# The second gate's products of a block in three bfloat16 parts instead of float32 (attention, a top-1 expert layer and a capacity expert layer on one core)

## What is computed

```python
attn = local_and_global_attention(q, k, v)            # 4 x 8 heads, 768 positions, 64 wide
x = attn rows                                          # 3072 tokens x 512
# first expert layer: one expert per token, only where x @ w_skip > 0
e = argmax(x @ moe_w_gate); g = softmax(x @ moe_w_gate)[e]
x[live] += g * (relu(x @ moe_w1[e]) @ moe_w2[e])       # 8 experts, 512 -> 1024 -> 512
# second expert layer: tokens are assigned by the sorted second gate's logits, at most 384 per expert
logits2 = x @ moe2_w_gate                              # 3072 x 8
assign greedily in falling order of logits2
out = relu(x @ moe2_w1[e]) @ moe2_w2[e]
```

## Time and profile before

| | |
|---|---|
| Time, median of 3 runs | 813.74 us (812.87 to 814.51) |
| Profiled execution's own time | 815.21 us |
| Its span in the trace | 813.5 us |
| TensorE matmul busy | 753.9 us, 93% of the span |
| VectorE busy | 537.1 us, 66% |
| ScalarE busy | 453.7 us, 56% |
| GpSimd (POOL) busy | 165.4 us, 20% |
| First experts in the trace | about 246 to 470 us |
| Mean granted clock of TensorE | 0.97 |

### The profile page before, as it was taken

The page is one execution under the profiler, slowest core; times in us unless marked ns, Lnnn a source line. Parts: engine busy times, 40 slices in busy tenths (PEclk is TensorE's granted clock), DMA queues, the critical chain, the costliest instruction groups (busy, mean ns, idle before and its releaser), DMA issues. The chain is left out here.

```text
span 813.5 us, 15742 instructions
## 1 busy us (share of the span) xinstructions
PE 753.9 (93%) x5590; PEld 675.1 (83%) x5590; DVE 537.1 (66%) x1463; ACT 453.7 (56%) x919; POOL 165.4 (20%) x184
## 2 busy tenths in 40 slices
PE   2899999999959999999999938999999999999997
PEld 2899999999928988899888825888888888888896
DVE  6877778777477778766666557766666767675420
ACT  3889888888525454554545303545554554536360
POOL 8100000000030222222221101141414141423321
PEclk9999999999959999999999957999999999999999
DMA  8998987986264666535763006768675777769861
GB/s 179 217 215 221 240 204 210 212 209 167 99 205 156 215 241 216 182 121 218 245 223 126 13 9 227 186 223 199 198 199 194 196 208 187 220 178 302 226 130 44
DMA packets 64106, 151.65 MB, mean 186 GB/s; under 512 B 12294, under 2 KB 15750, under 8 KB 64016
## 3 DMA queue, kind: packets, MB, share of 16 engines
q1 hardware_dynamic: 52512, 114.77, 48.3%
q0 software_dynamic: 11504, 35.72, 18.1%
HBM read 118.84 MB, written 16.67 MB: 167 GB/s over the span
## 5 line engine op out<-in xcount | busy, mean ns | idle before, releaser
L1817 PE MATMUL r_ph<-r_xh,r_w1h 128*128 128x384 f32 x256 | 90.6, 354 | 0.0
L1817 PE MATMUL r_ph<-r_xh,r_w1l 128*128 128x384 f32 x256 | 86.2, 337 | 0.0
L1817 PE MATMUL r_ph<-r_xl,r_w1h 128*128 128x384 f32 x256 | 85.8, 335 | 0.0
L592 ACT ACTIVATE pr<-pr,nmx 128x232 f32<-128x232 f32 (+1 forms) x192 | 79.9, 467 | 9.6 <-DVE nmx L685 9.6
L1098 PE MATMUL m_ph<-m_xh,m_w1h 128*128 128x224 f32 x288 | 80.9, 281 | 0.1
L1252 ACT ACTIVATE m_hh<-m_ph 128x224 fp32r<-128x224 f32 (+1 forms) x72 | 25.2, 350 | 97.9 <-PE m_ph L1098 93.9
L1098 PE MATMUL m_ph<-m_xh,m_w1l 128*128 128x224 f32 x288 | 79.1, 275 | 0.0
L1098 PE MATMUL m_ph<-m_xl,m_w1h 128*128 128x224 f32 x288 | 78.9, 274 | 0.0
L685 DVE CUSTOM_DVE_ANT_0 pr<-sc,bias 128x232 f32<-128x232 f32 (+1 forms) x192 | 65.0, 374 | 19.5 <-PE sc L466 17.5
L599 ACT ACTIVATE prt<-tp 128x384 f32<-128x384 f32 (+1 forms) x128 | 65.5, 537 | 22.0 <-PE tp L478 18.5
L1831 PE MATMUL r_py<-r_w2h,r_hh 128*128 128x512 f32 x192 | 76.1, 396 | 0.0
(11 more groups left out here) (298 smaller groups left out, 1960.5 us busy)
## 6 DMA issues: line engine op xcount, KB each, us to landing
r_w<-moe_w SPq DMA_DIRECT2D x64, 512.0 KB, 5.1
m_w<-moe_w SPq DMA_DIRECT2D x36, 512.0 KB, 5.9
row_buf<-moe_w SPq DMA_DIRECT2D x9, 2048.0 KB, 8.7
r_w2l<-r_w POOLq DMA_DIRECT2D x32, 512.0 KB, 4.9
k_raw<-kI SPq DMA_DIRECT2D x64, 208.0 KB, 7.2
q_raw<-qT SPq DMA_DIRECT2D x64, 192.0 KB, 7.6
vo<-vL SPq DMA_DIRECT2D x16, 384.0 KB
x_rows<-row_buf SPq DMA_DIRECT2D x4, 1536.0 KB, 6.6
```

Of the source, the lines that this page charges most:

```text
L592: nc.scalar.activation(pr[n % PRS][:, t, lo:CW], pr[n % PRS][:, t, lo:CW], ACT.Exp, bias=nmx[n % PRS][:, t:t + 1], scale=-1.0).then_inc(ex ...
L1817: last = nc.tensor.matmul(ph[m % 4][:, 0:CAP], w[:, c, m * P:(m + 1) * P], x[:, c, :], start=(c == 0 and a == 0), stop=(c == KC - 1 and a ...
```

## The change

The second gate's products of blocks 0 to 7 no longer read float32 rows and weights. The weights are split once into three bfloat16 parts (`split_gate2`, in VectorE's side work of block 0), which lie side by side as 24 columns. The turned rows of a block are split into three bfloat16 parts too: ScalarE writes the first (its copy now goes to `y_parts[0]`), VectorE subtracts it from the turned rows into `yt` (float32), ScalarE writes the second from `yt` for two chunks at once, and VectorE subtracts again into the third. All nine products are taken by 24 matmuls with 24 moving columns, accumulated over chunks and row parts, and VectorE sums the three groups of 8 columns. `Z_AT` becomes 2, 3, 4, 5: the wide copies and subtractions stand behind chunks 3 and 4, the products behind chunk 5 as before. TensorE's turns of chunk 2 and 3 now wait for VectorE's subtraction (`yt_low`) of chunk 0 and 1. The overflow block's own gate part stays float32.

```diff
+        wg2_parts, wg2_rest = sb("wg2_parts", [P, KC, 3, E], BF16), sb("wg2_rest", [P, KC, E])
+            y_parts = [tb(f"y_part{i}", [P, KC, WIDE1], BF16) for i in range(3)]
-            Z_AT, OVER_AT = (2, 3, 5), 3
+            Z_AT, OVER_AT = (2, 3, 4, 5), 3
+            def in_parts(k):
+                return isinstance(k, int) and k < E
+            def kept_before(k):
+                return 6 * k if isinstance(k, int) and k <= E else KC * k + (6 - KC) * E
 # TensorE, z_part
                             if c >= 2:
-                                pe.wait_ge(yt_kept, KC * k + c - 1)
+                                pe.wait_ge(yt_low if in_parts(k) else yt_kept, kept_before(k) + c - 1)
-                    else:
-                        pe.wait_ge(yt_kept, KC * k + KC)
+                    elif i == 3 and in_parts(k):
+                        pe.wait_ge(yt_kept, kept_before(k) + 6)
+                        pe.wait_ge(yt_low, kept_before(k) + 6)
                         for t in tiles(k):
                             r = rows_in(k, t)
                             for c in range(KC):
-                                last = nc.tensor.matmul(pt[0][0:r, BLK + t * E:BLK + (t + 1) * E], yt[:, c, t * P:t * P + r], wg2[:, c, :],
-                                                        start=(c == 0), stop=(c == KC - 1))
+                                for a in range(3):
+                                    last = nc.tensor.matmul(pt[0][0:r, BLK + t * 3 * E:BLK + (t + 1) * 3 * E], y_parts[a][:, c, t * P:t * P + r],
+                                                            wg2_parts[:, c].rearrange("p a e -> p (a e)"), start=(c == 0 and a == 0), stop=(c == KC - 1 and a == 2))
+                        last.then_inc(z_done, 1)
 # ScalarE, z_part
-                            nc.scalar.activation(yt[:, c, 0:W], pt[c % 2][:, BLK:BLK + W], ACT.Copy).then_inc(yt_kept, 1)
+                            dst = y_parts[0][:, c, 0:W] if in_parts(k) else yt[:, c, 0:W]
+                            nc.scalar.activation(dst, pt[c % 2][:, BLK:BLK + W], ACT.Copy).then_inc(yt_kept, 1)
+                    if i in (1, 2) and in_parts(k):
+                        two = slice(2 * i - 2, 2 * i)
+                        act.wait_ge(yt_low, kept_before(k) + 2 * i)
+                        nc.scalar.activation(y_parts[1][:, two, :], yt[:, two, 0:WIDE1], ACT.Copy).then_inc(yt_kept, 1)
 # VectorE, z_part
+                    if i < 2 and in_parts(k):
+                        for c in (2 * i, 2 * i + 1):
+                            dve.wait_ge(yt_kept, kept_before(k) + c + 1)
+                            v.tensor_tensor(yt[:, c, 0:WIDE1], pt[c % 2][:, BLK:BLK + WIDE1], y_parts[0][:, c, :], ALU.subtract).then_inc(yt_low, 1)
+                    if i in (1, 2) and in_parts(k):
+                        two = slice(2 * i - 2, 2 * i)
+                        dve.wait_ge(yt_kept, kept_before(k) + 4 + i)
+                        v.tensor_tensor(y_parts[2][:, two, :], yt[:, two, 0:WIDE1], y_parts[1][:, two, :], ALU.subtract).then_inc(yt_low, 1)
-                            last = v.tensor_copy(zo[s][0:r, t, :], pt[0][0:r, BLK + t * E:BLK + (t + 1) * E])
+                                parts = pt[0][0:r, BLK + t * 3 * E:BLK + (t + 1) * 3 * E].rearrange("p (a e) -> p e a", e=E)
+                                last = v.tensor_reduce(zo[s][0:r, t, :], parts, AX.X, ALU.add)
 # VectorE, ahead of the rest of count_extra
+                def split_gate2():
+                    link(v.tensor_copy(wg2_parts[:, :, 0, :], wg2[:]))
+                    link(v.tensor_tensor(wg2_rest[:], wg2[:], wg2_parts[:, :, 0, :], ALU.subtract))
+                    link(v.tensor_copy(wg2_parts[:, :, 1, :], wg2_rest[:]))
+                    link(v.tensor_tensor(wg2_parts[:, :, 2, :], wg2_rest[:], wg2_parts[:, :, 1, :], ALU.subtract))
```

More of the change, by code:

```diff
@@ L848, in build @@
             h_done, h_high, h_low, y_done, y_kept = (sem(x) for x in ("h_done", "h_high", "h_low", "y_done", "y_kept"))
-            yt_turned, yt_kept, z_done, z_kept = (sem(x) for x in ("yt_turned", "yt_kept", "z_done", "z_kept"))
+            yt_turned, yt_kept, yt_low, z_done, z_kept = (sem(x) for x in ("yt_turned", "yt_kept", "yt_low", "z_done", "z_kept"))
             gathered, scattered, z_scattered = ([sem(f"{x}{s}") for s in range(2)] for x in ("gathered", "scattered", "z_scattered"))
@@ L1081, in z_part @@
                             for c in range(KC):
-                                last = nc.tensor.matmul(pt[0][0:r, BLK + t * E:BLK + (t + 1) * E], yt[:, c, t * P:t * P + r], wg2[:, c, :],
-                                                        start=(c == 0), stop=(c == KC - 1))
+                                for a in range(3):
+                                    last = nc.tensor.matmul(pt[0][0:r, BLK + t * 3 * E:BLK + (t + 1) * 3 * E], y_parts[a][:, c, t * P:t * P + r],
+                                                            wg2_parts[:, c].rearrange("p a e -> p (a e)"), start=(c == 0 and a == 0), stop=(c == KC - 1 and a == 2))
+                        last.then_inc(z_done, 1)
+                    elif i == 3:
+                        pe.wait_ge(yt_kept, kept_before(k) + KC)
+                        for c in range(KC):
+                            last = nc.tensor.matmul(pt[0][:, BLK:BLK + E], yt[:, c, 0:P], wg2[:, c, :], start=(c == 0), stop=(c == KC - 1))
                         last.then_inc(z_done, 1)
@@ L1176, in _ @@
                 with pe.If(n < 1):
-                    for i in range(3):
+                    for i in range(4):
                         z_part(E - 1, 1, i)
@@ L1195, in _ @@
                         turn_limits()
-                    z_part(E, 0, 2)
+                    z_part(E, 0, 3)
                     with pe.If(n < 2):
@@ L1312, in z_part @@
                 def z_part(k, s, i):
-                    if i == 2:
+                    if i < 2 and in_parts(k):
[6 more added lines that the diff above has]
+                        v.tensor_tensor(y_parts[2][:, two, :], yt[:, two, 0:WIDE1], y_parts[1][:, two, :], ALU.subtract).then_inc(yt_low, 1)
+                    if i == 3:
                         dve.wait_ge(z_done, k + 1)
@@ L1320, in z_part @@
                             r = rows_in(k, t)
-                            last = v.tensor_copy(zo[s][0:r, t, :], pt[0][0:r, BLK + t * E:BLK + (t + 1) * E])
+                            if in_parts(k):
+                                parts = pt[0][0:r, BLK + t * 3 * E:BLK + (t + 1) * 3 * E].rearrange("p (a e) -> p e a", e=E)
+                                last = v.tensor_reduce(zo[s][0:r, t, :], parts, AX.X, ALU.add)
+                            else:
+                                last = v.tensor_copy(zo[s][0:r, t, :], pt[0][0:r, BLK:BLK + E])
                         last.then_inc(z_kept, 1)
@@ L1432, in gates_of_slots @@
                     gates_from(gate_parts, SLOTS, gates1[:, 0:SLOTS]).then_inc(gated, 1)
+                def split_gate2():
[3 more added lines that the diff above has]
+                    link(v.tensor_tensor(wg2_parts[:, :, 2, :], wg2_rest[:], wg2_parts[:, :, 1, :], ALU.subtract))
                 def count_extra():
+                    split_gate2()
                     z_rows_of_slots()
```

## The result

The changed kernel takes 823.26 us (median of 4 runs, 821.95 to 826.86) against 813.43 us before (4 runs): 1.0121 times, 95% interval 1.0102 to 1.014.

What follows compares the result with a forecast made beforehand. TensorE, full in the first experts, was taken as the bound; 0.54 + 1.07 - 0.18 = 1.43 us per block over eight blocks, with 0.5 for irregularity, gave +11.8 us: 825.5 us, range 818.5 to 829.0.

Steps and rivals of the forecast that it cites:

- What bounds the stage: First experts: TensorE is busy in all 25.00 us of a block, so any wait put on it is paid whole.
- The first wait: Before the second transposes, TensorE waits for VectorE's subtraction, queued behind the low part of w2: 0.54 us per block.
- The second wait: Before the gate products, TensorE waits for VectorE's second wide subtraction, behind chunk 4's low parts: 1.07 us per block.
- The gate products: On TensorE, 24 bfloat16 matmuls take 1.32 us instead of 1.50 in float32: a gain of 0.18 us per block.
- Rival A: Gate products: 96-column loads as fast as 128-column ones, gain 0.78 us per block, kernel 820.9 us; chance 0.27.
- VectorE stays in step: VectorE's added 2.5 to 2.8 us per block fit; it is in step with TensorE again before chunk 6.
- Rival C: VectorE falls behind for good, so w2 products wait too, 0.5 to 1 us more per block: 830 to 834 us; chance 0.06.
- Irregularity: ScalarE's late starts on chunk 3, in two of eight blocks, partly reach the gate products: 0.5 us in all.
- Rival B: First experts: VectorE's new work is done before TensorE arrives, both waits summing below 0.18 us; chance 0.05.
- Rival D: First experts: the clock falls because TensorE pauses; one fall gives about 840 us; chance 0.02.
- the two signs that were named: Block start to start in the changed kernel: 26.4 us by the forecast, 25.8 us if Rival A holds.

Runs made afterwards that it cites:

- gate_first: The changed kernel with VectorE's gate subtractions ahead of, not behind, the low part of w2 of the same chunk: 816.91 us, ratio to before 1.0037.
- both_hidden: The changed kernel with the gate's parts behind hidden chunks 2, 4, 5 and 7 instead of 2, 3, 4 and 5: 808.11 us, ratio to before 0.9927.
- after_again2: The changed kernel itself, run again unchanged for a second profiled execution: 819.40 us.
- best_wide: both_hidden with the second tile's parts widened by zeros, so its products load 128 columns instead of 96: 806.35 us, ratio to before 0.9911.
- first_hidden: The changed kernel with the gate's parts behind hidden chunks 2, 4, 5 and 6: 826.55 us, ratio to before 1.0149.
- f32_products: The changed kernel with the gate's products in float32 as before, splitting and waits kept: block 26.74 us; its whole time, 1591.18 us, isn't comparable.

## Why the prediction was right, and where a term was off

**What bounds the stage.** Right. TensorE was full, and every wait put on it was paid whole: +8.7 us in the stage by the trace.

**The first wait.** Forecast 0.54 us from the earlier trace rows, measured 0.56: the transposes start 0.49 us later (0.34 us of it shows as idle time) and take 0.07 us longer, since chunk 3's two wait as well. Cause as told: gate_first takes VectorE's low part of w2 out from in front and the wait falls to 0.21; both_hidden removes it.

**The second wait.** Forecast 1.07, measured 1.20 (1.14 to 1.26 in the other full blocks, 1.07 in the overflow block). ScalarE starts chunk 4's high part at 8.28 us of the block (8.26 forecast) and VectorE ends at 10.48 (10.41); the other half is the way from VectorE's end to TensorE's start, 0.14 us where 0.06 had been taken from the earlier trace rows. One part of the account was too simple. The prediction put both waits down to the low part of w2 queued in front, and by the changed kernel's rows it is in front here too (385.57, then 386.17). But ScalarE's second wide copy ends at 385.93 us, only 0.24 us before that wide subtraction starts:

```profile
385.36 0.57 ACT L1267 ACTIVATE m_y_part<-m_yt 128x448 bf16<-128x448 f32 x1
```

Taking the low part of w2 away can't gain more than that, and in gate_first it shortened this wait by 0.20 us. What costs most is the way from chunk 4 through ScalarE.

**The gate products.** This is the term of the sum that was mis-sized. Forecast 1.32 us, a gain of 0.18; measured 0.84, a gain of 0.66. The wide loads came as forecast (25 ns in the trace; 30 taken). For the narrow ones the upper bound was taken, 80 ns, from the float32 loads; they take 45 (in after_again2 the 12 wide products of block 5 take 0.30 us and the 12 narrow ones 0.54). Rival A had 0.72 us for all, so it was nearer than the forecast, though its narrow loads aren't as fast as wide ones either. 0.48 us too much in eight blocks are 3.8 us: without them the forecast would have been 821.7. The Trainium skill ("TensorE: Matmul & The Clock Gate", "Weight-path perf modes — Fast Weight Load (FWL) and DoubleRow") says that only loads of 128 columns, of a type that isn't float32, are fast. The trace agrees in the order, 125 against 95 ns of one load, and best_wide shows it: filling up to 128 columns saves 0.24 us per block. What failed was to read the other side of the rule as "as slow as float32".

**VectorE stays in step.** Right: 1.55 us of idle time ahead of chunk 6 against 1.57 before. Rival C fell, and the transposes of the next block don't wait.

**Irregularity.** 0.5 us forecast. In the profiled execution one block (k = 4, 26.50 us) is 0.4 longer than its neighbours, by 0.72 us of idle time ahead of the second transposes instead of 0.34. The size was right, the place wasn't: ScalarE is late there at hidden chunk 1 (3.79 us into the block; 2.88 in others), as it was in the same block before at no cost (3.69). Late starts on chunk 3, of which the prediction spoke, occur in blocks 2, 5 and 6 and cost at most 0.1 us each. In the two later executions no block is late.

**Rival B, not slower.** It would have taken both waits below the gain. With the same instructions two and one chunks later that is both_hidden: 0.9927. What decided was the distance in TensorE's list between the split and its use, not the work.

**Rival D, the clock.** Not seen in the three profiled executions of the changed kernel, but the margin is small: in first_hidden a pause 0.2 us longer went with a fall in five of seven blocks, and in f32_products the same pause with longer products behind it went with one in four. Its price was badly wrong: a fall costs 1.6 us, at most 3.3, not about 14. And the attention stage was weak evidence: it isn't full of pauses. From 100 to 150 us TensorE is busy for 48.95 of 50 us, and from 40 to 225 us it waits 15 times, 4.8 us in all and 1.1 us at most.

**The sum.** 0.56 + 1.20 - 0.66 = 1.10 us against 1.43 forecast per block. The measured time lies in the range; by mechanism the forecast's two waits held, by size it is rival A with slightly longer waits. That 823.26 us fell into the forecast's own part of the range (822.5 to 829) and not into A's (818.5 to 822.5) is luck. The stage's own +8.7 us give 822.1, and the later comparison gave 820.46. The block, 26.09 us, lies between the two signs that were named (26.4 and 25.8).

## What to carry to other kernels

Before work is split among engines to shorten the bound engine's part, ask what the new inputs wait for and how many of its own instructions lie between: here the products lost 0.66 us a block and gained 1.76 us of waiting, and moving them one or two chunks back in the list turned +1.2% into -0.7%. A place counts for every engine in the chain: the second wait went through ScalarE's copy as much as through VectorE's queue. Price a wait by the whole queue ahead of the producing instruction, with the other operand's work in it. For bfloat16 weights fill tiles up to 128 columns where room is left.

## What the runs showed of the hardware that was not expected

- A bfloat16 load of 96 columns takes 125 ns and sets 45 ns from product to product; one of 128 columns takes 95 and sets 25. In float32 it is 165 ns for 96 columns and 192 for 128.
- TensorE started 0.14 us behind the end of the VectorE instruction that released it within a full stream, 0.06 us at the end of the overflow block.
- The granted clock fell from 1.00 to 0.50 (2.4 to 1.2 GHz) in a stage that was otherwise full, behind 1.26 us of standing still and 0.84 us of small products (first_hidden, five of seven blocks). Each of these falls cost 1.6 us; in f32_products two cost 3.3. Filling the pause with products that nobody reads kept the clock up and gained some 8 us.
